# Sliding-window attention with the values as the stationary operand, division after a second transposition, and the router's sums taken head by head

## The chip, the cores and the metric

## The reference

Three stages run one after the other. The attention stage has 2 batches, 8 heads, 768 tokens and 64 columns a head. A token attends to the first 8 keys and to the 96 keys up to itself, with a linear bias for distance:

```
scores = q k^T / 8 - slope[h] * dist ;  a = exp(scores - max) ;  a = a / (sum(a) + 1e-9)
x = concat over heads of (a v)                                   # 2 x 768 x 512
```

The router stage takes `logits = x w_gate` (8 experts) and a gate column `x w_local`. A token whose local gate is below 0.5 takes the best expert, any other takes the expert of the token before it. The token then goes through the two matrices of its expert (512 to 1024 to 512, with a ReLU between them), scaled by its softmax probability.

The mixing stage is a 2-D Fourier transform over tokens and columns, its real part added to the input, a layer norm, and a dense 512 to 2048 to 512 network.

## The kernel before

The kernel is written by hand for each engine with semaphores: the text of an engine is its order of work. The changed part is the attention stage, the branch `windowed > 0`.

**Units.** A unit is one tile of 128 tokens of one pair of heads: 2 batches x 4 pairs x 6 tiles is `UNITS` = 48 units. Unit n belongs to group g = n // 6 (a batch and a pair of heads) and tile i = n % 6. A unit has up to two key tiles of 128 keys for each head (`k` = 0, 1); the first tile of a group (i = 0) has one.

**Loop of TensorE.** Iteration n issues, in this order: `scores(n+2)` (two products of 64 rows with 256 columns, one for each head, on different row halves), `turn(n)` (four transpositions of the probabilities into `prob_t`'s bank), at some steps `turn_x`, at some steps tasks of the router, and then `values(n-1)`. `values` holds a tile of transposed probabilities as the stationary operand and passes 128 columns of the values by it: four products, 8 records, into bank 6. It waits for `x_unit_done`, because VectorE has to have read bank 6.

**Loop of VectorE.** Iteration n: every sixth time `bias_of` (two operations), `scores(n+2)` (scale, bias and maximum, two operations), `turned(n)` (copy of the transposed probabilities out of PSUM), in odd iterations `reciprocals`, at some steps half a piece of `first_rest` (the low part of the first expert's weights), at twelve steps from `STEP_FLAGS` = 34 on a part of the router's work for batch 0 (`stages`: the first of each pair reads bank 6 and waits for `pv_done`, the second stands behind the division), and `normalised(n-1)`, which divides bank 6 into `x_att`.

**Loop of ScalarE.** Iteration n: `exponentials(n+2)` (two Exp, each with its sum), at some steps `copy_x` (transposed x out of bank 7 into `x_t`), and at every fourth step `first_expert` (the high part of a piece of the first expert's weights, 128x1024).

**Router sums.** `turn_x` transposes finished tiles of `x_att` (48 transpositions over the loop), `copy_x` copies them to `x_t`, and `gate_sums` multiplies a tile of `x_t`, held still, by 9 columns of `gate_w`: 48 products for both batches. Batch 0's (`sum_logits`) are tasks of iterations 28 to 33, eight records each. Those of batch 1 are taken in three parts in iterations 40 to 47 and behind the loop.

**After the loop.** `take_logits(1)` on VectorE starts a serial chain: the choice of expert for batch 1, ranks, slots, scatter of x by GpSimd's indirect DMA, load of the sorted tiles by SP. Then TensorE runs the experts and the mixing stage almost without a pause to the end.

**DMA.** SP issues the first loads in one order: `cwin`, keys, `square`, values, `gate_w`, the first weight piece, zeros, then the keys and values of the following groups.

## Time and profile before

| | us |
|---|---|
| median of 3 runs | 662.52 (660.62 to 666.81) |
| the profiled execution, as timed | 663.25 |
| its span in the trace | 661.4 |
| TensorE matmul busy | 641.9 (97%) |
| TensorE weight load busy | 523.3 (79%) |
| VectorE busy | 314.8 (48%) |
| ScalarE busy | 210.0 (32%) |
| GpSimd busy | 213.5 (32%) |

The granted clock of TensorE is 9 tenths or more in all 40 slices, that is 2.4 GHz throughout. PE stands for TensorE's matmuls, PEld for its weight loads, DVE for VectorE, ACT for ScalarE, POOL for GpSimd, SPq for the DMA issues of SyncE. A record of a matmul spans its whole way through the array and overlaps the next one, so the pace of a series is read from start to start and not from the duration.

### The profile page before, as it was taken

How to read it: one execution, taken by the hardware profiler on the slowest of the kernel's cores; microseconds unless marked ns; L12 is line 12 of the kernel's file. 1: busy time of each engine (PE TensorE's matmuls, PEld its weight loads, DVE VectorE, ACT ScalarE, POOL GpSimd, SP SyncE). 2: the span in 40 equal slices, each digit the busy share in tenths (PEclk: the TensorE clock that was granted, in tenths of full speed). 3: DMA queues.
4: the chain of work that ended last, by engine and by line, in shares of the span. 5: the costliest groups of instructions: out<-in, count | busy, mean ns of one | idle time of the engine just before them, and what ended most of it. 6: DMA issues, size and time to landing. Idle time of an engine off the chain costs nothing. (4 is left out here: it accounts for less than half of the span.)

```text
span 661.4 us, 10419 instructions
## 1 busy us (share of the span) xinstructions
PE 641.9 (97%) x3346; PEld 523.3 (79%) x3347; DVE 314.8 (48%) x830; ACT 210.0 (32%) x414; POOL 213.5 (32%) x120
## 2 busy tenths in 40 slices
PE   9999999889999999999998999999999999999997
PEld 7777878768888888887776778888888888888886
DVE  5999787476744544634546864521121112211112
ACT  3566544222444243342215552232111122111110
POOL 0000000233999787987436465340000000000000
PEclk9999999999999999999999999999999999999999
DMA  8897543323777755866444054100010000100001
GB/s 319 301 324 256 209 143 118 113 84 126 249 237 234 264 202 182 282 238 197 151 124 125 1 175 143 35 30 1 1 64 1 0 1 1 63 1 0 1 1 63
DMA packets 36486, 83.71 MB, mean 127 GB/s; under 512 B 3286, under 2 KB 8150, under 8 KB 36440
## 3 DMA queue, kind: packets, MB, share of 16 engines
q1 hardware_dynamic: 19888, 43.34, 18.8%
q10 hardware_dynamic: 14632, 33.46, 15.0%
q0 software_dynamic: 1920, 6.29, 3.0%
q8 instruction: 29, 0.48, 0.3%
q14 instruction: 17, 0.14, 0.1%
HBM read 67.36 MB, written 15.73 MB: 126 GB/s over the span
## 5 line engine op out<-in xcount | busy, mean ns | idle before, releaser
L782 POOL TENSOR_TENSOR w<-raw,w 128x1024 fp32r<-128x1024 f32 x56 | 132.6, 2398 | 26.9 <-ACT w L881 26.9
L1881 DVE SCALAR_TENSOR_TENSOR act_t<-psum,act_t 128x512 fp32r<-128x512 f32 x48 | 33.2, 691 | 190.1 <-ACT act_t L1180 190.1
L881 ACT ACTIVATE w<-raw 128x1024 fp32r<-128x1024 f32 x64 | 67.4, 1058 | 97.2 <-POOL w L782 31.6
L1180 ACT ACTIVATE act_t<-psum 128x512 fp32r<-128x512 f32 x48 | 28.8, 599 | 216.2 <-PE psum L620 216.2
L618 PE MATMUL psum<-un_t,wc 128*128 128x512 f32 x192 | 74.8, 390 | 1.4 <-DVE un_t L1808 1.4
L618 PE MATMUL psum<-wc,act_t 128*128 128x512 f32 x192 | 75.6, 394 | 0.0
L620 PE MATMUL psum<-wc,act_t 128*128 128x512 f32 x192 | 74.9, 390 | 0.0
L619 PE MATMUL psum<-wc,act_t 128*128 128x512 f32 x192 | 74.8, 390 | 0.0
L620 PE MATMUL psum<-un_t,wc 128*128 128x512 f32 x192 | 74.7, 389 | 0.0
L619 PE MATMUL psum<-un_t,wc 128*128 128x512 f32 x192 | 74.7, 389 | 0.0
L954 ACT ACTIVATE prob<-prob,top 128x256 f32<-128x256 f32 (+1 forms) x96 | 46.3, 482 | 51.5 <-DVE top L1521 47.9
L790 POOL DMA_INDIRECT x_sorted<-x_att,slots x12 | 11.8, 987 | 134.7 <-DVE slots L1367 131.6
L618 PE MATMUL psum<-w,xs_t 128*128 (+1 forms) x128 | 52.1, 407 | 1.3 <-POOL w L782 1.0
L618 PE MATMUL psum<-w,hid_t 128*128 (+1 forms) x128 | 51.6, 403 | 0.8 <-DVE hid_t L1684 0.8
L2112 PE MATMUL psum<-v_win,prob_t 128*128 128x128 f32 x352 | 49.2, 281 | 1.8 <-DVE x_att L1549 1.7
L620 PE MATMUL psum<-w,xs_t 128*128 (+1 forms) x128 | 50.2, 392 | 0.0
L620 PE MATMUL psum<-w,hid_t 128*128 (+1 forms) x128 | 50.1, 391 | 0.0
L619 PE MATMUL psum<-w,hid_t 128*128 (+1 forms) x128 | 49.9, 390 | 0.0
L619 PE MATMUL psum<-w,xs_t 128*128 (+1 forms) x128 | 49.8, 389 | 0.0
L862 POOL TENSOR_TENSOR wc<-raw,wc 128x1024 fp32r<-128x1024 f32 x15 | 35.7, 2402 | 31.6 <-ACT wc L1130 24.4
L2112 PEld LDWEIGHTS psum<-v_win,prob_t 128*128 128x128 f32 x352 | 43.0, 192 | 3.5 <-issue 3.4
L618 PEld LDWEIGHTS psum<-un_t,wc 128*128 128x128 f32 x192 | 36.1, 188 | 9.1 <-DVE un_t L1808 1.6
(289 smaller groups left out, 1099.4 us busy)
## 6 DMA issues: line engine op xcount, KB each, us to landing
raw<-in_moe_w ACTq DMA_DIRECT2D x56, 512.0 KB, 4.3
raw<-in_moe_w_ch SPq DMA_DIRECT2D x12, 512.0 KB, 3.3
k_win<-in_k SPq DMA_DIRECT2D x7, 768.0 KB, 7.6
v_win<-in_v SPq DMA_DIRECT2D x7, 704.0 KB, 5.2
xs<-x_sorted SPq DMA_DIRECT2D x17, 256.0 KB, 4.2
raw<-in_moe_w SPq DMA_DIRECT2D x8, 512.0 KB, 8.5
y_sorted<-ys SPq DMA_DIRECT2D x16, 256.0 KB, 3.6
out<-u SPq DMA_DIRECT2D x12, 256.0 KB, 2.0
```

Source lines behind the costliest of these rows:

```text
L618: nc.tensor.matmul(target, left_h, right_h, start=first, stop=False)
L619: nc.tensor.matmul(target, left_h, right_l, start=False, stop=False)
L620: return nc.tensor.matmul(target, left_l, right_h, start=False, stop=last)
L782: nc.gpsimd.tensor_tensor(w[:, slot, 1, m, at_:at_ + PIECE], raw[:, n % RING, :], w[:, slot, 0, m, at_:at_ + PIECE].bitcast(f32), ALU.subt ...
L790: pool.indirect_dma_start(x_sorted[:, :], bass.IndirectOffsetOnAxis(ap=slots[:, t:t + 1], axis=0), x_att[:, t, :], None).then_inc(first_sc ...
L862: nc.gpsimd.tensor_tensor(lo, source, hi.bitcast(f32), ALU.subtract).then_inc(wc_ready, 1)
L881: nc.scalar.activation(w[:, slot, 0, m, at_:at_ + PIECE], raw[:, n % RING, :], ACT.Copy).then_inc(high_done, 1)
L954: ins = nc.scalar.activation(prob[n % 3][:, t, c0:], prob[n % 3][:, t, c0:], ACT.Exp, bias=top[:, n % 3, t:t + 1], scale=-1.0, accum_out=s ...
L1180: nc.scalar.activation(act_t[n % 2][:, 0, :], bank(act_bank(n)), ACT.Relu).then_inc(act_high, 1)
L1881: nc.vector.scalar_tensor_tensor(act_t[n % 2][:, 1, :], bank(act_bank(n)), 0.0, act_t[n % 2][:, 0, :].bitcast(f32), ALU.max, ALU.subtract) ...
L2112: ins = nc.tensor.matmul(bank(6)[:, t * D:t * D + P], prob_t[n % 2][:, 2 * t + k, :], v_flat[r][:, at_:at_ + P], start=(k == k0), stop=(k ...
```

## The change

- `values(n)` holds a tile of the values still (`v_win`) and passes both heads' probabilities by it as 256 columns: two products (4 records) of 256 columns in place of four (8 records) of 128. Bank 6 then holds both heads' values by both heads' probabilities with the head's columns on the partitions; the two quarters that belong together are used. `OVER`, the place of the router's results in bank 6, moves behind the 256 columns.
- ScalarE copies the two quarters into `x_pair` (two copies of 64 partitions x 128 columns a unit, `copy_pair(n-1)` in iteration n, behind `exponentials(n+2)` and ahead of `first_expert`). `values(n)` on TensorE now waits for `pair_copied`, no longer for the division.
- TensorE turns `x_pair` back to tokens (`turn_pair(n-2)` in iteration n, between `turn(n)` and `values(n-1)`: one transposition into bank 7), and multiplies the same tile, held still, by `gate_pair`: 18 columns, the router's 9 sums for each of the two heads.
- VectorE divides from bank 7 (`normalised(n-2)` in iteration n) and once in a group multiplies the group's gate sums by the reciprocals into `by_head`. `add_heads` adds over heads: over 8 in a stage of its own for batch 0, over 6 at iteration 45 for batch 1; `take_logits(1)` adds the last two with two operations.
- `turn_x`, `copy_x`, `sum_logits`, `sum_part`, `sum_third`, `sum_last` leave this branch.
- `STEP_FLAGS` is 28 in place of 34, with one stage more at its head; the bank-reading stages wait for `pair_copied` in place of `pv_done`. `PIECE_STEPS` is every fifth step in place of every fourth.
- One DMA more: `gate_pair` (72 columns, 36 KB) behind `gate_w` on SP's queue, and TensorE waits for both before iteration 0.

The diff, cut to its core (the other branch and the declarations are left out):

```diff
@@ -555,28 +567,24 @@
             return 5 - n % 2
-        X_FILLS = []
-        for g_ in range(B * HP - 2):
-            X_FILLS += [(6 * g_ + 9, g_, 0, 4), (6 * g_ + 10, g_, 4, 2)]
-        X_FILLS += [(41, 6, 0, 4), (43, 6, 4, 2), (45, 7, 0, 2), (47, 7, 2, 2), (UNITS, 7, 4, 2)]
+        X_FILLS = [(g_, t0, n) for g_ in range(B * HP) for t0, n in ((0, 4), (4, 2))]
         def x_fills_for(g, t):
-            return 1 + [t0 <= t < t0 + n and g_ == g for _, g_, t0, n in X_FILLS].index(True)
-
-        PIECE_STEPS = {4 * i + 3: i for i in range(WPIECES)}
-
-        SUM_STEP = {ST * HP + 4 + t: t for t in range(ST)}
-        PART_STEP = {40 + t: t for t in range(ST)}
-        THIRD_STEP = {42 + t: t for t in range(ST)}
-        PART_TAKEN = 46
-        LAST_STEP = 47
-        STEP_FLAGS = 34
+            return 2 * g + 1 + t // 4
+
+        PIECE_STEPS = {5 * i + 3: i for i in range(WPIECES)}
+
+        PART_TAKEN = 45
+        STEP_FLAGS = 28
         small = bank(6)
-        OVER = P + D
+        OVER = 2 * P
         BANK_LOGITS, BANK_PART = (small[:, P + OVER + n * ST * (E + 1):P + OVER + (n + 1) * ST * (E + 1)]
                                   for n in range(2))
         BANK_LAST = bank(7)[:, 2 * P:2 * P + ST * (E + 1)]
+        BANK_PAIR = [bank(7)[:, m * P:(m + 1) * P] for m in range(2)]
+        BANK_GATED = [bank(7)[:, 2 * P + n * 2 * ST * (E + 1):2 * P + (n + 1) * 2 * ST * (E + 1)]
+                      .rearrange("p (i t e) -> p i t e", i=ST, t=2) for n in range(2)]
         BANK_FLAGS = small[0:ST, 2 * P:4 * P]
         BANK_KEEP, BANK_FRESH = small[0:ST, 2 * P:3 * P], small[0:ST, 3 * P:4 * P]
         BANK_ENDS = small[0:1, OVER:OVER + 2 * ST]
...
@@ -657,6 +665,8 @@
                 first_group_keys(p)
                 first_group_values(p)
             sp.dma_start(gate_w[:, :, :], a["gate"]).then_inc(gate_loaded, 16)
+            sp.dma_start(gate_pair[:, :, :, :].rearrange("p c t e -> p (c t e)"),
+                         a["gate_pair"].rearrange("p c t e -> p (c t e)")).then_inc(gate_loaded, 16)
             def first_piece(n):
                 sp.dma_start(raw[:, n, :], w1_d[:, 0:1, n, :].rearrange("p e f -> p (e f)")
                              ).then_inc(raw_loaded[n], 16)
...
@@ -956,19 +966,28 @@
                                                    accum_out=sums[:, n % 4, t:t + 1])
                     ins.then_inc(prob_ready, 1)
+                def copy_pair(n):
+
+                    act.wait_ge(pv_done, n + 1)
+                    if n >= 3:
+                        act.wait_ge(pair_turned, n - 2)
+                    for t in range(2):
+                        rows = slice(t * D, (t + 1) * D)
+                        ins = nc.scalar.activation(x_pair[rows, n % 3, :], bank(6)[rows, t * P:(t + 1) * P], ACT.Copy)
+                    ins.then_inc(pair_copied, 1)
+
                 exponentials(0)
                 exponentials(1)
                 for n in range(UNITS):
                     if n + 2 < UNITS:
                         exponentials(n + 2)
-                    for k, fill in enumerate(X_FILLS):
-                        if fill[0] == n:
-                            copy_x(k)
+                    if n > 0:
+                        copy_pair(n - 1)
                     if n in PIECE_STEPS:
                         first_expert(PIECE_STEPS[n])
-                    if n == STEP_FLAGS + 1:
+                    if n == STEP_FLAGS + 2:
                         gate_exponentials(0)
-                copy_x(len(X_FILLS) - 1)
+                copy_pair(UNITS - 1)
             with nc.scalar.Else():
                 with act.Fori(0, B * HP) as group:
                     for v in range(2 * ST):
...
@@ -1251,15 +1270,20 @@
             def take_logits(b):
+                flat = logits[:, :, :].rearrange("p t e -> p (t e)")
                 if b == 0:
                     dve.wait_ge(logit_sums, ST)
-                    nc.vector.tensor_copy(logits[:, :, :].rearrange("p t e -> p (t e)"), BANK_LOGITS
-                                          ).then_inc(logits_ready, 1)
+                    nc.vector.tensor_copy(flat, BANK_LOGITS).then_inc(logits_ready, 1)
                 else:
-                    dve.wait_ge(last_sums, ST)
-                    nc.vector.tensor_tensor(logits[:, :, :].rearrange("p t e -> p (t e)"), BANK_LAST,
-                                            logits_part[:, :, :].rearrange("p t e -> p (t e)"), ALU.add
+                    link(nc.vector.tensor_tensor(logits_part[:, :, :], logits_part[:, :, :], by_head[:, :, H - 2, :],
+                                                 ALU.add))
+                    nc.vector.tensor_tensor(logits[:, :, :], logits_part[:, :, :], by_head[:, :, H - 1, :], ALU.add
                                             ).then_inc(logits_ready, 1)
+
+            def add_heads(into, heads):
+                return nc.vector.tensor_reduce(into[:, :, :],
+                                               by_head[:, :, 0:heads, :].rearrange("p t h e -> p t e h"),
+                                               AX.X, ALU.add)
             def below_top(b):
                 dve.wait_ge(logits_ready, b + 1)
...
@@ -1537,21 +1561,31 @@
                 def reciprocals(n):
                     both = slice((n - 1) % 4, n % 4 + 1)
-                    nc.vector.tensor_scalar(inv[:, both, :], sums[:, both, :], 1e-9, None, ALU.add
+                    kept = inv_all[:, n - 1:n + 1, :]
+                    nc.vector.tensor_scalar(kept, sums[:, both, :], 1e-9, None, ALU.add
                                             ).then_inc(sums_eps, 1)
                     dve.wait_ge(sums_eps, (n + 1) // 2)
-                    nc.vector.reciprocal(inv[:, both, :], inv[:, both, :]).then_inc(inv_ready, 1)
+                    nc.vector.reciprocal(kept, kept).then_inc(inv_ready, 1)
                 def normalised(n):
                     g, i = n // ST, n % ST
-                    dve.wait_ge(pv_done, n + 1)
+                    dve.wait_ge(pair_turned, n + 1)
                     dve.wait_ge(inv_ready, n // 2 + 1)
+                    if i == ST - 1:
+                        nc.vector.tensor_tensor(
+                            by_head[:, :, 2 * (g % HP):2 * (g % HP) + 2, :], BANK_GATED[g % 2],
+                            inv_all[:, g * ST:(g + 1) * ST, :].unsqueeze(3).broadcast_to([P, ST, 2, E + 1]), ALU.mult
+                            ).then_inc(pair_gated, 1)
                     nc.vector.tensor_tensor(
                         x_att[:, (g // HP) * ST + i, (g % HP) * P:(g % HP + 1) * P].rearrange("p (t d) -> p t d", t=2),
-                        bank(6)[:, 0:P].rearrange("p (t d) -> p t d", t=2),
-                        inv[:, n % 4, :].unsqueeze(2).broadcast_to([P, 2, D]), ALU.mult).then_inc(x_unit_done, 1)
-
-                stages = ((take_logits, below_top), (None, best_codes), (None, choose_fresh),
+                        BANK_PAIR[n % 2].rearrange("p (t d) -> p t d", t=2),
+                        inv_all[:, n, :].unsqueeze(2).broadcast_to([P, 2, D]), ALU.mult).then_inc(x_unit_done, 1)
+
+                def sum_heads(b):
+                    dve.wait_ge(pair_gated, HP)
+                    add_heads(logits, H).then_inc(logits_ready, 1)
+
+                stages = ((None, sum_heads), (None, below_top), (None, best_codes), (None, choose_fresh),
                           (take_flags, run_in_tiles), (take_ends, run_over_tiles), (all_codes, None),
                           (hot_codes, None), (take_counts, rank_all), (None, place), (None, areas),
                           (None, share_sums), (None, share))
...
@@ -1573,19 +1607,19 @@
                     reads_bank, behind = stages[n - STEP_FLAGS] if 0 <= n - STEP_FLAGS < len(stages) else (None, None)
                     if reads_bank is not None:
-                        dve.wait_ge(pv_done, n)
+                        dve.wait_ge(pair_copied, n)
                         reads_bank(0)
+                    if n > 1:
+                        normalised(n - 2)
                     if n == PART_TAKEN:
-                        dve.wait_ge(pv_done, n)
-                        take_part()
-                    if n == LAST_STEP:
-                        dve.wait_ge(pv_done, n)
-                        take_third()
-                    if n > 0:
-                        normalised(n - 1)
+                        dve.wait_ge(pair_gated, 2 * HP - 1)
+                        add_heads(logits_part, H - 2).then_inc(part_ready, 1)
                     if behind is not None:
                         behind(0)
+                normalised(UNITS - 2)
                 normalised(UNITS - 1)
+                dve.wait_ge(part_ready, 1)
+                dve.wait_ge(pair_gated, 2 * HP)
                 chain_end, chain[0] = chain[0], chain_start
             with nc.vector.Else():
                 dve.wait_ge(g_dist, 16)
...
@@ -2095,58 +2134,52 @@
                     g, i, r = n // ST, n % ST, n // ST % 2
                     k0 = 1 if i == 0 else 0
                     pe.wait_ge(prob_t_ready, n + 1)
-
-                    if g == 0 and i == 0:
-                        pe.wait_ge(first_values[0], VALUES_FIRST)
-                    if g == 0 and i % 2 == 1 and i < ST - 1:
-                        pe.wait_ge(first_values[i // 2 + 1], VALUES_FIRST)
+                    if g == 0 and i % 2 == 0:
+                        pe.wait_ge(first_values[i // 2], VALUES_FIRST)
                     if g > 0 and i == 0:
                         pe.wait_ge(v_loaded[r], (VALUES_FIRST if r == 0 else 16) + 16 * (g // 2))
                     if n > 0:
-                        pe.wait_ge(x_unit_done, n)
+                        pe.wait_ge(pair_copied, n)
                     for task in tasks:
                         task()
-                    for t in range(2):
-                        for k in range(k0, 2):
-                            at_ = (2 * i + k - 1) * P + t * D
-                            ins = nc.tensor.matmul(bank(6)[:, t * D:t * D + P], prob_t[n % 2][:, 2 * t + k, :],
-                                                   v_flat[r][:, at_:at_ + P], start=(k == k0), stop=(k == 1))
+                    for k in range(k0, 2):
+                        ins = nc.tensor.matmul(bank(6)[:, 0:2 * P], v_win[r][:, 2 * i + k - 1, :],
+                                               prob_t[n % 2][:, k:4:2, :], start=(k == k0), stop=(k == 1))
                     ins.then_inc(pv_done, 1)
+
+                def turn_pair(n):
+                    g, i = n // ST, n % ST
+                    pe.wait_ge(pair_copied, n + 1)
+                    if n > 0:
+                        pe.wait_ge(x_unit_done, n)
+                    nc.tensor.transpose(BANK_PAIR[n % 2], x_pair[:, n % 3, :], ident)
+                    nc.tensor.matmul(BANK_GATED[g % 2][:, i, :, :].rearrange("p t e -> p (t e)"), x_pair[:, n % 3, :],
+                                     gate_pair[:, g % HP, :, :].rearrange("p t e -> p (t e)"), start=True, stop=True
+                                     ).then_inc(pair_turned, 1)
                 scores(0)
                 scores(1)
                 warm_up(4)
                 pe.wait_ge(square_loaded, 16)
                 pe.wait_ge(v_padded, 2)
-                by_step = {STEP_FLAGS + 3: turn_flags, STEP_FLAGS + 4: ends_to_row, STEP_FLAGS + 5: carry_to_column,
-                           STEP_FLAGS + 6: codes_to_columns, STEP_FLAGS + 7: rank_tokens}
+                pe.wait_ge(gate_loaded, 2 * 16)
+                by_step = {STEP_FLAGS + 4: turn_flags, STEP_FLAGS + 5: ends_to_row, STEP_FLAGS + 6: carry_to_column,
+                           STEP_FLAGS + 7: codes_to_columns, STEP_FLAGS + 8: rank_tokens}
                 for n in range(UNITS):
                     if n + 2 < UNITS:
                         scores(n + 2)
                     turn(n)
-                    for k, (step_, g, t0, size) in enumerate(X_FILLS):
-                        if step_ == n:
-                            pe.wait_ge(x_unit_done, g * ST + t0 + size)
-                            turn_x(k)
+                    if n > 1:
+                        turn_pair(n - 2)
                     tasks = []
-                    if n in SUM_STEP:
-                        tasks.append(lambda t=SUM_STEP[n]: sum_logits(t))
                     if n in by_step:
                         tasks.append(lambda stage=by_step[n]: stage(0))
-                    if n in PART_STEP:
-                        tasks.append(lambda t=PART_STEP[n]: sum_part(t))
-                    if n in THIRD_STEP:
-                        tasks.append(lambda t=THIRD_STEP[n]: sum_third(t))
                     if n > 0:
                         values(n - 1, tasks)
-                for t in (2, 3, 0, 1):
-                    sum_last(t)
+                turn_pair(UNITS - 2)
                 values(UNITS - 1)
-                pe.wait_ge(x_unit_done, UNITS)
-                turn_x(len(X_FILLS) - 1)
                 turn_tile(0, 0, 16)
-                for t in range(4, ST):
-                    sum_last(t)
+                turn_pair(UNITS - 1)
                 keep_busy(5, bank(0))
             with nc.tensor.Else():
                 pe.sem_inc(g_x, 1)
```

## Rows read from the trace of the kernel before

**Rows 1.** The page: the span, and busy time of each engine.

```profile
span 661.4 us, 10419 instructions
PE 641.9 (97%) x3346; PEld 523.3 (79%) x3347; DVE 314.8 (48%) x830; ACT 210.0 (32%) x414; POOL 213.5 (32%) x120
```

**Rows 2.** Windows: stretch, length, then busy (records) of PE, PEld, DVE, ACT, POOL.

```profile
10.78:70.96 60.18, 58.42 (x433) 44.90 (x432) 54.74 (x214) 38.48 (x130) 0.00 (x0) 1.00 0.87 311
70.96:121.01 50.05, 48.78 (x386) 40.34 (x386) 39.25 (x165) 23.17 (x82) 5.05 (x5) 1.00 0.40 142
121.01:132.17 11.16, 8.40 (x64) 7.40 (x63) 4.71 (x18) 2.25 (x7) 0.97 (x1) 1.00 0.22 74
132.17:661.40 529.23, 516.49 (x2411) 421.64 (x2409) 211.04 (x413) 144.12 (x193) 206.32 (x104) 1.00 0.31 102
```

**Rows 3.** Timeline of PE, one plain unit: start, length, line, count of records.

```profile
33.75 0.70 PE L2079 MATMUL psum<-k_win,q_t 64*128 64x256 f32 x4
34.39 0.66 PE L2090 MATMUL psum<-square,prob 128*128 128x128 f32 x4
34.88 1.06 PE L2112 MATMUL psum<-v_win,prob_t 128*128 128x128 f32 x8
35.87 0.70 PE L2079 MATMUL psum<-k_win,q_t 64*128 64x256 f32 x4
```

**Rows 4.** Timeline of PE: filler products of 256 fp32 columns, each with its weight load.

```profile
130.91 2.40 PE L1985 MATMUL psum<-square 128*128 128x256 f32 x10
...
148.67 4.05 PE L1985 MATMUL psum<-square 128*128 128x256 f32 x18
```

**Rows 5.** Groups by line (count, busy, mean ns), and eight gate loads of the timeline.

```profile
L2112 PE MATMUL psum<-v_win,prob_t 128*128 128x128 f32 x352 | 49.2, 281 | 1.8 <-DVE x_att L1549 1.7
...
80.79 0.97 PEld L1933 LDWEIGHTS psum<-gate_w,x_t 128*128 128x128 f32 x8
```

**Rows 6.** Groups of ACT by line and shape: copies out of PSUM, shorter Exp.

```profile
L954 ACT ACTIVATE prob<-prob,top 128x128 f32<-128x128 f32 x16 | 6.3, 394 | 9.8 <-DVE top L1521 9.6
...
L916 ACT ACTIVATE x_t<-psum 128x512 f32<-128x512 f32 x7 | 4.0, 574 | 0.0
L916 ACT ACTIVATE x_t<-psum 128x256 f32<-128x256 f32 x10 | 3.7, 368 | 7.0 <-PE psum L1927 6.1 <-remote 0.9
```

**Rows 7.** Timeline of all engines, 78 to 83 us: who follows whom.

```profile
78.70 1.14 PE L2112 MATMUL psum<-v_win,prob_t 128*128 128x128 f32 x8
...
79.77 0.70 PE L2079 MATMUL psum<-k_win,q_t 64*128 64x256 f32 x4
...
79.88 0.29 DVE L1549 TENSOR_TENSOR x_att<-psum,inv 128x128 f32<-128x128 f32 x1 [1.03 <-PE psum L2112]
...
80.52 0.42 DVE L1521 CUSTOM_DVE_ANT_0 prob<-psum,pair_bias 128x256 f32<-128x256 f32 x1 [0.35 <-PE psum L2079]
...
81.33 0.51 ACT L954 ACTIVATE prob<-prob,top 128x256 f32<-128x256 f32 x1 [1.70 <-DVE top L1521]
...
82.33 1.04 ACT L881 ACTIVATE w<-raw 128x1024 fp32r<-128x1024 f32 x1
```

**Rows 8.** DMA: issue of `gate_w` and of the first piece; `gate_w` to landing.

```profile
6.12 0.44 SPq L659 DMA_DIRECT2D gate_w<-in_gate  x1
...
6.60 0.45 SPq L661 DMA_DIRECT2D raw<-in_moe_w  x1
...
DMA to landing us min/median/max: 5.5/5.5/5.5
```

**Rows 9.** Group of DVE by line and shape: a router step on six partitions.

```profile
L1316 DVE TENSOR_TENSOR_SCAN kept_all<-flags_t,zeros 6x128 f32<-6x128 f32 x2 | 0.8, 386 | 0.0
```

**Rows 10.** Timeline of the end of the attention stage.

```profile
123.88 0.36 PE L1933 MATMUL psum<-gate_w,x_t 128*128 128x9 f32 x2 [2.27 <-DVE prob_t L1535]
...
129.18 0.29 DVE L1549 TENSOR_TENSOR x_att<-psum,inv 128x128 f32<-128x128 f32 x1 [1.31 <-PE psum L2112]
...
132.17 0.21 DVE L1260 TENSOR_TENSOR logits<-psum,logits_part 128x54 f32<-128x54 f32 x1 [2.70 <-issue]
```

23 lines of the change are left out of this document (18 added, 5 removed).

## Prediction

> **What bounds the kernel now.** I read the page first [rows 1]: TensorE's matmul rows cover 97% of the span, VectorE 48%, ScalarE 32%. The windows [rows 2] split this. The loop over 48 units runs from 10.78 to 121.01, its end with the chain to the logits of batch 1 to 132.17, and then 529 us follow in which TensorE is 98% busy and which the change doesn't touch. They move as a whole with the moment of those logits, so only the first 132 us are to be costed. In the first window of the loop (28 units, 60.18 us, 2.15 a unit) VectorE is 91% busy and TensorE idle for 1.8; in the second (18 units, 50.05 us, 2.78 a unit) VectorE is at 78%, TensorE idle for 1.3, and the router's sums are what has been added. TensorE's order of work sets the pace, with VectorE close behind in the first window.
>
> A plain unit shows TensorE's ledger by starts [rows 3]: scores 33.75 to 34.39 (0.64), four transpositions to 34.88 (0.49, of which 0.11 is the first load of the series behind it), eight records of `values` to 35.87 (0.99), in all 2.12.
>
> **The values.** Eight records of 128 columns take 0.99, that is 0.124 each [rows 3]. Records of 256 fp32 columns follow one another at 0.21 with their loads hidden: 18 take 4.05 and 10 take 2.40, so eight more cost 1.65 [rows 4]. Four of them are 0.85 us. Gain: 0.13 a unit, 0.11 where there is one key tile (half the records, estimate); 40 x 0.13 + 8 x 0.11 = 6.1 us over the loop.
>
> The Trainium skill ("Perfetto Trace Analysis", Identifying the Most-Contended Engine) says to judge TensorE's headroom by its weight loads' busy time and not by the matmuls'. By that rule halving the loads would be the gain, and it is a rival below.
>
> **What moves on TensorE.** Transpositions: 48 before, 48 after, nothing. Gate sums: 48 products of 96 records before and after, each bound by its load, 0.11 to 0.12 (eight loads in 0.97 [rows 5]; eight records from 80.90 to the next `values` at 0.1 each). But they move: before, 80 of the 96 records stood in the second window and none in the first; now every unit has 2, 0.22 us. So the ledger per window changes like this. First window, 28 units: +28 x (0.22 - 0.13) = +2.5. Second, 18 units: -80 x 0.11 + 18 x 0.22 - 18 x 0.13 - some 4 transpositions x 0.11 = -7.6.
>
> **ScalarE's copies.** Two copies of 64 x 128 out of PSUM a unit. Rows of 256 and 512 columns take 368 and 574 ns [rows 6]: 0.8 ns a column and 162 ns fixed, so 0.27 for 128 columns, start to start 0.18, both finished 0.45 after the first starts. Lower bound 0.16 each (the fixed part), upper bound 0.39, the Exp of 128 columns [rows 6]; I take 0.27, since those rows are Copy out of PSUM too. ScalarE's load goes from 38.5 to about 50 in the first window: room enough. They lie on a path, though, worked out from [rows 7]. From TensorE's scores (79.77) to VectorE's is 0.75, from there to the first Exp 0.81, both Exp until ScalarE is free 1.00 (81.33 to 82.33), copies 0.45, wake-up 0.06: `pair_copied` comes 3.07 after the iteration's start. `values` started 1.46 after it and is visible 1.08 later (its four records, and the 0.2 by which 79.88 follows the last of the eight of 78.70), at 2.54, just before the Exp are over. `turn_pair` wants it after one period (0.64 + 0.38 + 0.33 + 0.11 + 0.85 = 2.31) and 1.02 more, at 3.33. So a plain unit costs nothing, with 0.26 us to spare. Iterations with one key tile are shorter on TensorE, and one in six waits about 0.1; a VectorE that is late (bias together with half a weight piece, twice in this window) costs 0.5 each time. Waits of the first window after the change: 5 x 0.1 + 2 x 0.5 = 1.5.
>
> Its waits before: six units have a ledger of 6 x 2.12 + 6 x 0.11 for transpositions, less 0.21, 0.22 and 0.45 for the short scores, turn and values (estimates, half of the long ones), 12.5 or 2.08 a unit; 28 x 2.08 less 1.4 for the first units, which have no `values` and no transposition yet, is 56.8, and 60.18 - 56.8 = 3.4 are waits, 1.8 of them plain idle [rows 2]. They come from divisions that VectorE does late, behind its wait for `values(n-1)`. That wait goes: it now divides n-2 out of another bank, and the unit of 2.17 gives it more time. So 56.8 + 2.5 + 0.2 (two transpositions more) + 1.5 = 61.0: **+0.7**. Bounds: -0.8 (no waits) and +5 (half of the late moments of VectorE reach TensorE).
>
> **The five reading stages.** This is the largest term. `take_flags` to `take_counts` (iterations 32 to 36) now wait for `pair_copied(n)`, which stands behind `exponentials(n+2)`, which waits for `scores(n+2)` of VectorE in the same iteration. That closes a ring: VectorE's scores, +0.81 Exp, +1.00, +0.45 copies, +0.06, then the stage, the division, what stands behind it, and only then `scores(n+3)`. One turn is 2.32 + stage + 0.25 + behind. Operations on six partitions cost about 0.39 [rows 9], small ones 0.2 to 0.25 (the 0.21 of [rows 10] and a link). So: flags 2.32 + 0.45 + 0.25 + 0.75 = 3.75; ends 3.1; codes 2.95; hot codes 2.85; counts, with four linked operations behind, 3.9: 16.5 against 5 x 2.17 = 10.9, +5.7. Before, the same stages waited for `pv_done`, without ScalarE in the ring. Around them VectorE is overloaded: `sum_heads` to `choose_fresh` at 29 to 31 together with a weight piece and reciprocals (+1), `place` (1.1 us in an odd iteration) and `share_sums` with bias and a piece (+2). All together +8; less the 0.3 of slack and the 0.7 that TensorE's own idle of 1.3 loses: second window -7.6 + 7.0 = **-0.6**, bounds -7.6 and +4.
>
> **The start.** TensorE now waits for `gate_pair` before iteration 0. SP issues it where the first piece stood, at 6.60, and the transfer before it took 5.5 to land [rows 8], so 12.1 against 10.78: **+1.3**. Lower bound 0.8 (landing in 5.0), upper bound 2.5. The DMAs behind it come 0.45 later; keys of group 1, issued at about 9, are not needed before 19: nothing.
>
> **The end.** From the start of iteration 46 (121.0) each `values` now follows the last through copy and `turn_pair`: 1.08 + 0.45 + 0.06 + 0.11 + 0.33 = 2.03. `values(45)` at +1.15, (46) +3.15, (47) +5.15, `turn_pair(47)` +6.75, seen at +7.3, gate product and division to +7.85. Before, the division of unit 47 began at 129.18, that is +8.2 with a wait of 2.27 before it that no row explains [rows 10]. VectorE then leaves the loop's branch: 2.70 idle until 132.17 though the last sums were there at 131.1 [rows 10]. If that is the cost of the branch's end, it is now fully exposed: +7.85 + 2.7, and one addition more, 0.25: 10.8 against 11.2, **-0.4**. Bounds: -2.0 (only 1.1 of it repeats), +1.9 (a wait of 2.3 as before comes again).
>
> **Sum.** +0.7 - 0.6 + 1.3 - 0.4 = +1.0. The profiled span was 661.4, its run 663.25, the median of three 662.52, 1.1 above the span. So 662.5 + 1.0 = **663.5**. Runs of this kernel can't tell a change under 1% (6.6 us) from none; this is one.
>
> **Rivals.**
> 1. *TensorE's ledger is paid out.* The reading ring doesn't bite, because the stages' work hides in the wait. For it: VectorE's busy falls from 91 to 78% in the second window. Against it: the ring holds only in-order steps that all have rows. It gives 663.5 - 7.5 = 656; with the end at its lower bound 654. Chance 0.14.
> 2. *The copies close a ring in every unit* (slower). If a copy costs 0.39 as the short Exp, the pair ends 0.24 later, and the 0.26 to spare is gone. From there every lateness of VectorE, some 0.25 a unit, goes to TensorE: 40 x 0.22 = 9 us, 672. It decides from 0.40 a copy on, or from 0.25 us of mean lateness. For it: `copy_pair` stands in order behind Exp that wait for VectorE, and VectorE is at 91% in the first window. Against it: rows of copies out of PSUM. Chance 0.21.
> 3. *The loads were the bound.* 176 loads of `values` fewer at 0.12 [rows 5] are 21 us: 641. Against it: fillers of 256 columns go at 0.21 a record [rows 4], though their one load would fit twice into it nearly, so the columns set their pace. By the rule quoted above the loads would set it. Chance 0.02.
>
> My forecast has 0.63, with a range of its own of 659 to 668. The range over all reaches to 656 and to 671. Faster by over 1%: rival 3 and most of rival 1, 0.13. Slower by over 1%: most of rival 2, 0.19. The rest, 0.68, is no change.
>
> **What the changed kernel's profile would show.** Records of `values` at 0.21 from start to start, a plain unit of 2.3; copies of 0.27; the first `scores` of the loop 1.3 later. The first window's 28 units should take about 61, the next 18 units 49.5 with periods of 2.9 to 3.9 in iterations 32 to 36, where VectorE's reading operation waits for ScalarE's copy. A copy of 0.4, many waits of TensorE's `x_pair` load for ScalarE, or periods of 2.3 in iterations 32 to 36 would make this wrong, as would a different cost of the branch's end.

## The result, and the profile after

| | before | after |
|---|---|---|
| median, us | 662.77 (660.62 to 666.81, 4 runs) | 675.25 (672.93 to 677.23, 4 runs) |
| the profiled execution, its span | 661.4 | 670.8 |
| TensorE matmul busy | 641.9 | 645.1 |
| TensorE weight load busy | 523.3 | 510.6 |
| ScalarE busy | 210.0 | 230.5 |

After is 1.018 of before, 95% interval [1.0121, 1.0238]: some 12 us slower, where 1 was forecast and 671 was the upper end of the range.

The windows of after, cut at the same iterations as [rows 2] (stretch, length, then busy and records of PE, PEld, DVE, ACT and POOL, the granted clock, DMA share, GB/s). The first is iterations 0 to 3, which had no window of their own before:

```profile
12.19:21.22 9.03, 9.03 (x47) 5.62 (x47) 6.05 (x26) 5.12 (x19) 0.00 (x0) 0.81 1.01 402
21.22:78.08 56.86, 56.36 (x345) 38.17 (x344) 47.84 (x191) 43.18 (x150) 0.00 (x0) 1.00 0.75 256
78.08:129.69 51.61, 45.06 (x273) 29.89 (x273) 42.06 (x178) 32.03 (x114) 6.45 (x6) 1.00 0.43 154
129.69:141.10 11.41, 8.43 (x47) 6.36 (x45) 3.86 (x13) 2.50 (x10) 0.00 (x0) 1.00 0.01 4
140.00:144.00 4.00, 0.83 (x3) 0.36 (x4) 2.74 (x12) 1.05 (x3) 0.00 (x0) 0.77 0.02 6
144.00:148.00 4.00, 3.51 (x13) 1.79 (x13) 1.56 (x8) 0.00 (x0) 0.00 (x0) 0.50 0.00 0
148.00:152.00 4.00, 3.72 (x11) 3.14 (x12) 2.88 (x15) 0.00 (x0) 0.51 (x1) 0.50 0.00 0
152.00:156.00 4.00, 3.48 (x17) 2.50 (x15) 0.90 (x4) 1.68 (x3) 3.08 (x4) 0.95 0.45 174
```

Iterations whose scores are those of a first tile (records of 64x128 in place of 64x256) mark every sixth iteration in both traces, so that the loss can be put in a ledger. The scores of iteration 4 start at 17.93 before and 21.22 after; those of iteration 28 at 70.96 and 78.08; `turn(46)` at 121.01 and 129.69; the flags' transposition behind the logits at 134.13 and 143.06; the first `hid` of the experts on ScalarE at 140.19 and 152.10.

| stretch | before | after | loss, us |
|---|---|---|---|
| to iteration 4 | 17.93 | 21.22 | +3.3 |
| 4 to 28 | 53.03 | 56.86 | +3.8 |
| 28 to 46 | 50.05 | 51.61 | +1.6 |
| 46 to the flags | 13.12 | 13.37 | +0.3 |
| flags to the first `hid` | 6.06 | 9.04 | +3.0 |
| sum | | | +11.9 |

The rest of the program, which the change leaves alone, took 518.7 in this execution of after and 521.2 in that of before, so the spans differ by only 9.4. In the other kernels of this study that do the same routing it took 519.2 to 524.7; that is scatter (last section), and the 11.9 is close to the 12.5 between the medians.

**A plain unit.** TensorE's timeline (start, length of the group, line, records), to be laid beside [rows 3]:

```profile
23.44 0.70 PE L2118 MATMUL psum<-k_win,q_t 64*128 64x256 f32 x4
24.07 0.66 PE L2129 MATMUL psum<-square,prob 128*128 128x128 f32 x4
24.56 0.29 PE L2155 MATMUL psum<-square,x_pair 128*128 128x128 f32 x1
24.69 0.29 PE L2156 MATMUL psum<-gate_pair,x_pair 128*128 128x18 f32 x2
24.83 1.11 PE L2146 MATMUL psum<-prob_t,v_win 128*128 128x256 f32 x4
25.87 0.49 PE L2118 MATMUL psum<-k_win,q_t 64*128 64x256 f32 x2
```

The unit takes 2.43, where 2.31 was forecast. The scores (0.63) and `turn` (0.49) stand as forecast, and transposition and gate product together (0.13 and 0.14) take less than the 0.33 of the forecast. But the four records of 256 columns take 1.04 from their first to the next scores, where eight of 128 took 0.99 and 0.85 was forecast. The reader sees here the error of the largest saving. An iteration with one key tile has half the records, and the difference of the two kinds gives their true pace:

```profile
29.48 0.68 PE L2146 MATMUL psum<-prob_t,v_win 128*128 128x256 f32 x2
30.09 0.49 PE L2118 MATMUL psum<-k_win,q_t 64*128 64x256 f32 x2
```

Two records take 0.61, four take 1.04: 0.215 a record, and 0.18 that the scores start later than that pace asks for, whatever the number. In the kernel before, eight took 0.99 [rows 3] and four took 0.54:

```profile
38.90 0.61 PE L2112 MATMUL psum<-v_win,prob_t 128*128 128x128 f32 x4
39.44 0.70 PE L2079 MATMUL psum<-k_win,q_t 64*128 64x256 f32 x4
```

That is 0.11 a record, and 0.09 beside it. Two records of 128 columns cost about the same as one of 256 (0.22 and 0.215). What sets the 0.11 can't be told from this: a weight load alone goes at nearly the same pace (eight gate loads in 0.97 [rows 5]).

**The start.** TensorE waits for `gate_pair` until 12.19 and then works at half clock, 1.2 GHz, for part of the next few us (granted clock 0.57 in 12 to 16 us), where before it began at 10.78:

```profile
12.19 1.04 PE L2118 MATMUL psum<-k_win,q_t 64*128 64x256 f32 x4 [1.92 <-issue]
13.16 0.69 PE L2129 MATMUL psum<-square,prob 128*128 128x128 f32 x2
13.77 1.23 PE L2118 MATMUL psum<-k_win,q_t 64*128 64x256 f32 x4
```

The same four records of scores take 1.23 here and 0.70 in the plain unit. The row names no releaser; in two other traces with the same wait (the second run of the changed kernel and the one with fewer gate products) it is the DMA of `gate_pair`.

**The ring.** TensorE's iteration 33 of after, with VectorE still in its 32nd (what released a step is in brackets):

```profile
90.08 0.70 PE L2118 MATMUL psum<-k_win,q_t 64*128 64x256 f32 x4
90.54 0.56 ACT L976 ACTIVATE x_pair<-psum 64x128 f32<-64x128 f32 x2
...
91.13 0.41 DVE L1335 COPY flags_t<-psum 6x256 f32<-6x256 f32 x1 [1.13 <-ACT x_pair L976]
91.57 0.29 DVE L1579 TENSOR_TENSOR x_att<-psum,inv_all 128x128 f32<-128x128 f32 x1
...
92.01 0.30 PE L2155 MATMUL psum<-square,x_pair 128*128 128x128 f32 x1 [0.64 <-DVE x_att L1579]
```

VectorE waits for the copies, the division follows, and TensorE's transposition waits for the division. The next scores follow at 93.87, a period of 3.79; the following three start after another 3.21, 3.52 and 3.02.

**A gap that not every execution has.** In iterations 41 and 42 both ScalarE (until 117.24) and VectorE (until 118.84) stand still for something that the trace calls only "remote" (rows of the waits of 20 to 130 us: total, times, longest):

```profile
DVE prob L1545 <- remote: 1.5, 1, 1.5
ACT x_pair L976 <- remote: 1.0, 1, 1.0
```

Iteration 40 to `turn(46)` takes 16.94 here. In the runs below with more fillers and with the last unit moved, whose loops up to there are the same, neither row is there and it takes 15.40 and 15.41. So 1.5 us of the 51.61 belong to this execution and not to the change. No run shows the cause.

**The end.** VectorE's last rows of the loop, and the first behind it, to be laid beside [rows 10]:

```profile
137.33 0.27 DVE L1575 TENSOR_TENSOR by_head<-psum,inv_all 128x108 f32<-128x108 f32 x1 [1.77 <-PE psum L2156]
137.52 0.28 DVE L1579 TENSOR_TENSOR x_att<-psum,inv_all 128x128 f32<-128x128 f32 x1
140.85 0.22 DVE L1278 TENSOR_TENSOR logits_part<-logits_part,by_head 128x54 f32<-128x54 f32 x1 [3.05 <-issue]
143.06 0.37 PE L1996 MATMUL psum<-square,keep_old 128*6 128x128 f32 x1 [3.52 <-DVE fresh L1319]
```

TensorE, whose five filler products (ten records) end at 139.54, is idle for 3.52, and the windows above show half clock from about 143 to 152. Before it was idle for 0.81 there, at full clock.

### The profile page after: what moved, and what is told of

The parts are those of the page before. It is cut to its first block, busy times and chain, and to the rows that moved or that the text cites. A ratio compares the mean times of both kernels' runs of the same rounds, so it can differ in the third digit from the quotient of the medians.

```text
span 670.8 us, 10221 instructions
## 1 busy us (share of the span) xinstructions
PE 645.1 (96%) x3170; PEld 510.6 (76%) x3171; DVE 316.0 (47%) x838; ACT 230.5 (34%) x493; POOL 214.3 (32%) x120
## 4 chain that ended last, share of the span: by engine, by line
PE 83%; DVE 8%; issue 4%; ACT 2%; DMA 1%; POOL 0%; another core or an unknown queue 0%; DVEq 0%; SPq 0%; ACTq 0%; POOLq 0%
PE psum L626 22%; PE psum L628 22%; PE psum L627 22%; PE psum L2146 4%; PE psum L2118 3%; PE psum L2129 2%; PE psum L2078 2%; DVE prob L1545 1%; PE psum L2155 1%; PE psum L2031 1%; ACT x_pair L976 1%; ACT prob L964 1%; PE psum L2320 1%; DVE prob_t L1559 1%; PE psum L2024 1%
## 5 line engine op out<-in xcount | busy, mean ns | idle before, releaser
L626 PE MATMUL psum<-w,xs_t 128*128 (+1 forms) x128 | 53.3, 417 | 0.1
L628 PE MATMUL psum<-w,xs_t 128*128 (+1 forms) x128 | 51.1, 400 | 0.0
L627 PE MATMUL psum<-w,xs_t 128*128 (+1 forms) x128 | 50.8, 397 | 0.0
L2146 PE MATMUL psum<-prob_t,v_win 128*128 128x256 f32 x176 | 49.7, 401 | 0.0
L1545 DVE CUSTOM_DVE_ANT_0 prob<-psum,pair_bias 128x256 f32<-128x256 f32 (+1 forms) x96 | 34.6, 399 | 16.6 <-PE psum L2118 14.2
```

Source lines behind the costliest of these rows:

```text
L626: nc.tensor.matmul(target, left_h, right_h, start=first, stop=False)
L627: nc.tensor.matmul(target, left_h, right_l, start=False, stop=False)
L628: return nc.tensor.matmul(target, left_l, right_h, start=False, stop=last)
L1545: ins = nc.vector.tensor_tensor_reduce(out=prob[n % 3][:, t, c0:], in0=bank(2 * (n % 2) + t)[:, c0:KW], in1=pair_bias[:, t, m0:m0 + KW - c ...
L2146: ins = nc.tensor.matmul(bank(6)[:, 0:2 * P], v_win[r][:, 2 * i + k - 1, :], prob_t[n % 2][:, k:4:2, :], start=(k == k0), stop=(k == 1))
```

## Experiments

All are edits of the changed kernel. A ratio is to the kernel before, run beside it on the same chip. The changed kernel itself, run again:

> The changed kernel unaltered, on the chip of the runs beside it, as their yardstick. Expected 1.018 times the kernel before, 674 to 677 us, with a span of 671 to 675; a clock at half between about 12 and 16 us and between about 140 and 152 us.

Measured 676.35 (673.26 to 681.18), 1.0191 [1.0117, 1.0264]. The scores of iteration 4 came at 22.76 (after: 21.22), since the half clock lasted longer, 0.50 in 12 to 16 and 0.67 in 16 to 20. From iteration 4 to 28 it took 56.85, and from the flags to `hid` 9.04, as in the first execution of the changed kernel, "after" from here on.

**The wait for `gate_pair` moved to where it is first read.**

```diff
                 pe.wait_ge(v_padded, 2)
-                pe.wait_ge(gate_loaded, 2 * 16)
...
                     pe.wait_ge(pair_copied, n + 1)
+                    if n == 0:
+                        pe.wait_ge(gate_loaded, 2 * 16)
```

> The changed kernel with the wait for the two gate tables moved from ahead of the loop to the first multiplication by them (iteration 2). Theory: the wait costs 1.4 us itself and, through TensorE's idle time of 1.9 us after which the clock was granted at half, some 1.9 more: 3.3 us less than the changed kernel, first scores of iteration 4 at about 18 in place of 21.2. Rival (only the wait counts, the slow first iterations have another cause, such as loads that share the DMA engines): 1.4 us less, and the records between 12 and 16 us stay slow.

**The wait kept, and twelve warm-up products ahead of it in place of four.**

> The changed kernel with the wait left ahead of the loop, but twelve warm-up products in place of four before it, so that TensorE is busy while it waits. Theory (the clock is half of the loss): the wait of 1.4 us stays, the clock stays at full, 1.5 to 2 us less than the changed kernel. Rival (the slow records come from the late tables or loads): no difference to the changed kernel.

Measured: 673.19 (1.014 [1.0063, 1.0216]) for the first and 673.21 (1.0133 [1.0077, 1.0189]) for the second, against 676.35 on the same chip. The scores of iteration 4 came at 18.02 and 20.12, against 22.76 and the 17.93 of before. With the warm-up products TensorE was idle for 0.38 ahead of the loop, in place of 1.92, and the clock stayed at 1.00:

```profile
12.19 0.70 PE L2118 MATMUL psum<-k_win,q_t 64*128 64x256 f32 x4 [0.38 <-issue]
```

So the start has two parts: the wait itself is 2.1 (20.12 less 18.02), and the half clock that it brings is 1.1 (in after) to 2.6 (in the run here). The late wait removes both. The ratios' intervals overlap; it is the traces that separate these. The half clock doesn't come every time: of the nine traces with this wait and four warm-up products, seven have it, behind 1.92 to 2.82 of idle time, and two don't, behind 1.11 (more fillers at the end) and 1.59 (other banks). Those two reach iteration 4 at 19.89 and 19.87, about where the twelve warm-up products do.

**Products of 256 columns split again into two of 128, the values still held.**

```diff
-                    for k in range(k0, 2):
-                        ins = nc.tensor.matmul(bank(6)[:, 0:2 * P], v_win[r][:, 2 * i + k - 1, :],
-                                               prob_t[n % 2][:, k:4:2, :], start=(k == k0), stop=(k == 1))
+                    for t in range(2):
+                        for k in range(k0, 2):
+                            ins = nc.tensor.matmul(bank(6)[:, t * P:(t + 1) * P], v_win[r][:, 2 * i + k - 1, :],
+                                                   prob_t[n % 2][:, 2 * t + k, :], start=(k == k0), stop=(k == 1))
```

> The changed kernel with each product of 256 columns taken apart into two of 128 (one per head), with the same result: 8 records and 8 weight loads a unit in place of 4 and 4. By the prediction's price (0.124 us for a record of 128 columns, 0.21 for one of 256) this costs 0.13 us a unit, 6 us more than the changed kernel. Theory now: the columns set the pace in both forms (0.11 and 0.215 a record) and what differs is the gap until the next scores, which is shorter after narrow records: 0 to 0.06 us a unit less, 0 to 3 us less in all. A unit's values, from their first record to the next scores, 0.99 in place of 1.04.

Measured 676.13, against 676.35 unsplit; 1.0161 [1.011, 1.0213]. Its unit, in the same view as above:

```profile
26.30 1.14 PE L2147 MATMUL psum<-prob_t,v_win 128*128 128x128 f32 x8
27.37 0.49 PE L2118 MATMUL psum<-k_win,q_t 64*128 64x256 f32 x2
...
31.00 0.69 PE L2147 MATMUL psum<-prob_t,v_win 128*128 128x128 f32 x4
31.62 0.49 PE L2118 MATMUL psum<-k_win,q_t 64*128 64x256 f32 x2
```

1.07 for eight and 0.62 for four, beside 1.04 and 0.61. Twice the records and twice the loads cost 0.01 to 0.03 a unit, and iterations 4 to 28 took 57.17 beside 56.85. This settles the price of the values: the fewer, wider records bring next to nothing. The Trainium skill ("Perfetto Trace Analysis", Identifying the Most-Contended Engine) judges TensorE's headroom by MFU (the share of its peak arithmetic that is used) and its weight loads' busy time. Here the loads' busy time fell by 12.7 us while the kernel became slower, and putting 176 loads back changed no time. As a price of a load, which is how the third rival used it, that busy time is of no use in this loop.

**Thirteen fillers at the end in place of five.**

> The changed kernel with thirteen filler products behind the loop in place of five, 3.4 us more of work that nobody waits for, ending before the flags of batch 1 are ready. Theory (the idle time of 3.5 us in which VectorE leaves the loop's branch costs a clock at half for the next 8 to 10 us): the clock stays at full, about 3 us less than the changed kernel. Rival (the chain there hangs on VectorE and not on TensorE's clock): no difference.

Measured 669.57, 1.0171 [1.0129, 1.0213]. The clock stays at 1.00 throughout 140 to 160, and from the flags to `hid` it takes 6.04 (139.94 to 145.98), as before the change (6.06), where after takes 9.04. The traces give the clock's price at the end as 3.0 us. The ratio hardly moves from the 1.0191 of the unaltered kernel on another chip, and with its interval it can't show the gain on its own.

**The copies of a unit ahead of the Exp.**

```diff
+                    if n > 0:
+                        copy_pair(n - 1)
                     if n + 2 < UNITS:
                         exponentials(n + 2)
-                    if n > 0:
-                        copy_pair(n - 1)
```

> The changed kernel with ScalarE's copies of unit n-1 ahead of the exponentials of unit n+2 instead of behind them. Theory (a ring: VectorE's scores, Exp, copies, the router stage that waits for the copies, the next scores): the Exp leave the ring, iterations 32 to 36 fall from 3.1 to 3.8 us to about 2.5 to 3.0, and the 18 units that took 51.6 us take about 47; 3 to 5 us less in all. Rival (VectorE's load by itself is what stretches these units, or the exponentials now come late): less than 1 us less, or more time.

Measured 674.22, 1.0209 [1.0179, 1.024]: no gain. The marks say why. Iterations 28 to 40 took 32.88 in place of 34.67, but 4 to 28 took 58.29 in place of 56.86: TensorE waited there for 2.0 in all, each time for the division, where it had waited for 0.4 for a copy. The likely reason is that the Exp now come late and everything behind them. The ring got only 0.35 shorter a turn (3.44 and 2.86 for iterations 33 and 34, where after has 3.79 and 3.21 for the same work). What TensorE still waits for in 78 to 130 is nearly all the division (the other 0.4 us are two waits for router steps):

```profile
PE psum L2155 <- DVE x_att L1579: 3.4, 8, 0.9
```

So there were two rings, one nearly as long as the other. Through Exp: scores, Exp, copies, stage, division. And without them: `values`, copies, stage, division, `turn_pair`, `values`. The prediction had only the first. Breaking it brings what lies between the two.

**The last gate product and division moved behind the end of VectorE's branch.** (The same lines, called after `If`/`Else` have joined; a semaphore is kept level for the general branch.)

> The changed kernel with VectorE's last gate product and division behind the end of the loop's branch instead of ahead of it, so that leaving the branch runs while unit 47 is still copied and turned. The other branch isn't kept right here. Theory (leaving the branch costs about 3 us wherever it stands, and was exposed): the logits of batch 1 come about 2.7 us earlier, TensorE's idle time there falls from 3.5 to under 1 us, the clock stays at full, so 5 to 6 us less in all. Rival (the 3.05 us are a wait of another kind, such as for the sums or for late instructions that any place meets): the gap moves along, no gain.

Measured 668.8, 1.0137 [1.0116, 1.0157]. VectorE is idle as long as before, but now while TensorE and ScalarE finish the last unit:

```profile
136.71 0.27 DVE L1531 TENSOR_TENSOR by_head<-psum,inv_all 128x108 f32<-128x108 f32 x1 [2.77 <-issue]
```

From `turn(46)` to the flags it takes 11.22, against 13.37 in after and 13.1 to 13.3 in the other traces with the old end and all gate products: 2.15 us less, where 2.7 was expected. (From iteration 40 it takes 26.63 against 30.31, but 1.5 of that is the gap of iterations 41 and 42, which this execution doesn't have.) The idle time belongs to leaving the branch, wherever the work stands; of its 2.77, 1.0 still comes behind the end of TensorE's last product of the unit, at 135.67. TensorE is idle for 1.37 in place of 3.52, the clock falls all the same (0.60 in 144 to 148), for a shorter time, and flags to `hid` takes 7.28.

**Late wait, copies first and the late last unit together.**

> The three repairs together: gate tables awaited at their first use, copies ahead of the exponentials, last division behind the branch. If the three causes are separate, the gains add: 3.2 (measured) + 4 + 5.5, 12 to 13 us less than the changed kernel, about 663 us or 0.998 of the kernel before. If they share a cause, less.

Measured 663.57, 1.0072 [1.0051, 1.0094], clock 1.00 in all of its span. That is some 8 us less than the changed kernel (1.0191), where 12 to 13 were expected. By the marks, against after, the start gave 3.0, the end 5.3 (11.03 to the flags and 6.06 to `hid`), and the copies 0.4 (58.29 and 32.89 for the two stretches) where 4 was expected. Here TensorE is idle for 1.32 ahead of the flags and the clock stays full, so the idle time alone doesn't say whether it falls.

**The router's results of batch 0 in other banks.** The kernel keeps ScalarE and VectorE out of one PSUM bank at a time: a stage that reads bank 6 stands behind the copies out of it. Now the results are put in the upper halves of banks 2 and 0, whose lower halves hold scores of the other parity (the fillers' output moves to bank 1):

```diff
-        BANK_FLAGS = small[0:ST, 2 * P:4 * P]
+        even, odd = (bank(2), small), (bank(0), small)
+        BANK_FLAGS = [x[0:ST, 2 * P:4 * P] for x in even]
...
-                        dve.wait_ge(pair_copied, n)
                         reads_bank(0)
...
                 for n in range(UNITS):
+                    if n - 1 in by_step:
+                        pe.wait_ge(x_unit_done, n - 2)
                     if n + 2 < UNITS:
                         scores(n + 2)
```

> The router's results of batch 0 are put in the unused halves of the scores' banks 0 and 2, which ScalarE never touches, so the reading stages of iterations 32 to 36 no longer wait for the copies; TensorE waits for their division before the next scores. Theory (these stages stand in a ring through values, copy, stage, division, turn back, of which copying first took away only one side): VectorE's waits for ScalarE's copies (4.1 us in 78 to 130 of the changed kernel) go, iterations 28 to 40 take 32 to 33 us in place of 34.7, the whole 1.5 to 2.5 us less than the changed kernel. Rival (VectorE's own load of 2.9 to 3.4 us in these iterations sets their length): 34 to 34.7 and less than 0.7 us in the whole.

Measured 671.64 (1.0107 [1.007, 1.0144]), against 676.92 (1.0141 [1.0074, 1.0207]) for the changed kernel beside it; the intervals overlap, and the marks decide. Iterations 28 to 40 took 32.22, within the 32 to 33 of the theory of the ring. VectorE waits for no copy any more in 78 to 130, where in after it waited for them for 4.1 in all. What it waits for is scores (and 1.6 for the gap of iterations 41 and 42, which this execution has):

```profile
DVE prob L1546 <- PE psum L2117: 4.2, 5, 1.3
```

So the ring cost 2.5 us in these iterations. 32.22 is also what the kernel before took for them (32.20: 70.96 to 103.16), though that had its batch-0 sums there as well.

**The gate product left out for groups 2 to 7.**

```diff
+                    if g < 2:
+                        ins = nc.tensor.matmul(BANK_GATED[g % 2][:, i, :, :] ...
```

> The gate product of turn_pair is left out for groups 2 to 7 (iterations 14 to 49), whose sums then repeat those of groups 0 and 1, so that the tokens go to other experts than in the reference. Theory (TensorE's order sets the pace, and two records of 0.11 a unit are 0.22 on it): iterations 14 to 28 take 14 x 0.22 = 3.1 us less, so 4 to 28 take 53.8 in place of 56.86; 28 to 46 about 2 less, as far as VectorE's own work lets it; the whole 4 to 6 us below the changed kernel. Rival (the products run under waits that come anyhow): 4 to 28 at 56.5 or more, the whole less than 1 us below.

Iterations 4 to 28 took 55.47 (23.09 to 78.56) in place of 56.85: 1.4 less where 14 x 0.22 = 3.1 was expected, and 28 to 40 took 34.41, 0.3 less. A unit without the product can take 1.99, but the next one then waits for a copy:

```profile
51.27 0.49 PE L2118 MATMUL psum<-k_win,q_t 64*128 64x128 f32 x4
51.69 0.66 PE L2129 MATMUL psum<-square,prob 128*128 128x128 f32 x4
52.19 0.27 PE L2155 MATMUL psum<-square,x_pair 128*128 128x128 f32 x1
52.30 1.03 PE L2146 MATMUL psum<-prob_t,v_win 128*128 128x256 f32 x4
53.26 0.70 PE L2118 MATMUL psum<-k_win,q_t 64*128 64x256 f32 x4
53.89 0.66 PE L2129 MATMUL psum<-square,prob 128*128 128x128 f32 x4
54.57 0.33 PE L2155 MATMUL psum<-square,x_pair 128*128 128x128 f32 x1
```

The transposition starts 0.50 after `turn` in the first unit and 0.68 in the second, where the copy it waits for ends at 54.52. With the product the same two units took 2.21 and 2.44. Both theories missed: the product is 0.22 on TensorE, but only 0.1 a unit comes back, since right beneath lies the path through Exp and copies that rival 2 described (waits of TensorE for copies in 44 to 78: 1.1, in after 0.4). Its whole time (692.16) can't be read, because the routing differs and the experts' part with it.

**The best of these together:** late wait, late last unit, other banks, Exp ahead of the copies.

> Gate wait late, last division behind the branch end and the router's results in banks 0 and 2, together, and the exponentials ahead of the copies as in the change. Theory: first scores of iteration 4 at 18.0; 4 to 28 in 56.9 (58.3 with copies first); 28 to 40 in 32.5; from the last unit to the flags as in the earlier combination; clock full at the end. 2 us less than that combination, so 1.004 of the kernel before (1.000 to 1.008). Rival (VectorE's load sets the reading iterations): 34.5 for 28 to 40 and 1.007 or more.

> The changed kernel unchanged, as a measure for the three others on this chip: 1.018 to 1.019 of the kernel before, iteration 4 to 28 in 56.9 and 28 to 40 in 34.7 us.

Measured: 666.24 (12 runs) and 1.0009 [0.9981, 1.0038] of before, beside the 676.92 of the changed kernel. Marks: iteration 4 at 18.32, 4 to 28 in 56.86, 28 to 40 in 32.22, 40 to the flags in 27.29, flags to `hid` 7.31 with the clock still at 0.64 in 138 to 142. Its time can't be told from that of the kernel before; `hid` comes 1.8 us later (142.00 against 140.19). The 3.8 us of the first window are all still there, and the shorter end (27.29 against the 30.97 of before) pays for most of them; of those 30.97, 2.27 are the wait in iteration 46 that the prediction found no row for, so how much the change itself gains there is open. A kernel faster than before wasn't found.

## Why the prediction was wrong, step by step

**First window, +0.7 forecast: wrong by the price of the values.** The step that failed is "Eight records of 128 columns take 0.99, that is 0.124 each" [rows 3]. Dividing a series' time by its number put the gap ahead of the next scores into the pace, while the fillers' 0.21 [rows 4] was a pace taken between two series of different length. The same subtraction on the values gives 0.11 for 128 columns, that is the 0.21 of 256, and no gain. Without the saving of 28 x 0.13 = 3.6, the +0.7 of the 28 iterations becomes +4.3, that is 3.7 for the 24 from iteration 4 on, and +3.8 was measured in those. Two smaller errors go against each other: transposition and gate product took 0.27 and not 0.33, and the four wide records stand 0.18 and not 0.09 ahead of the scores. TensorE's idle time fell to 0.50 (56.86 less 56.36), from 1.74 in the same iterations before.

**The copies: right in size, their waits too high.** Two took 0.56 as a group of one engine, done 0.59 after the first starts at the stage that waits for them (90.54 to 91.13), where 0.51 was forecast. In the first window TensorE waited for them once, 0.4 in all, where the sum had 1.5 of waits. Rival 2 was wrong as a price of the change, but its ring lies just below, as the run with fewer gate products showed. Cheaper values would then have come back only in part as well; that is argued, no run made the values cheaper.

**The reading ring: right in place and nearly in size.** Periods of 3.79, 3.21, 3.52 and 3.02 of TensorE's iterations 33 to 36 (VectorE's 32 to 35) stand beside forecast turns of 3.75, 3.1, 2.95 and 2.85; bias and a weight piece in the third were counted apart. The turn with the counts, forecast at 3.9, came as 2.31 and then 3.88, the linked operations falling into the next one. The window took 51.61 where 49.45 was forecast; without 18 x 0.13 = 2.3 of the values the forecast would have been 51.8. That these agree is partly luck: 1.5 of the 51.61 is the gap of iterations 41 and 42, which nobody forecast, and without it the same loop took 50.06 and 50.07, so the other terms of this window were 1.7 too high. That ScalarE was its only cause was too simple, as the copies put first showed; moving the results to another bank took it away.

**The start: the wait right, its consequence missed.** Forecast 12.1, measured 12.19 (11.94 to 12.90 in the other traces with this wait). That TensorE is idle for 1.92 there, and then runs at half clock, was not in the sum: +3.3 at iteration 4, not +1.3. Of the 2.0 missed, 0.9 are the wait itself (with the clock full, iteration 4 comes 1.9 to 2.2 behind the kernel before) and 1.1 the half clock.

**The end: right in length, its consequence missed.** The branch end, taken as 2.70 and fully exposed, measured 3.05, and the stretch to the flags +0.3 against -0.4. But with the branch end exposed, TensorE's fillers run out 3.5 us ahead of the next product, and the clock falls to half for some 9 us: +3.0.

So, of the 10.9 us between the forecast (+1.0) and the ledger (+11.9), 5.5 are the values (42 units of 0.13), 2.0 the start, 3.0 the clock at the end and 0.7 the stretch to the flags; the second window came out 0.2 better than the corrected forecast, or 1.7 better and 1.5 worse by the gap.

## What to carry to other kernels

Take the pace of a series of matmuls from two series of different length, never from one series divided by its number; here that alone turned a saving of 6 us into none. Where a change puts a wait on TensorE, look at what the engine does just before and behind it, and price the work behind at both clocks. When a ring of waits is broken, look for the next one through the same buffers before counting the gain; in this loop two rings lay within 0.35 us a turn.

## What the runs showed of the hardware

**Leaving this branch leaves VectorE idle for 2.6 to 3.1 us.** 2.70 before, 3.05 after, 2.77 with a unit moved behind it. In twelve of the fourteen traces (2.70 to 3.05) no releaser is named; in the two combinations the rows of 2.72 and 2.61 name a record of TensorE. In the two gaps looked at (129.4 to 132.2 before, 137.5 to 141 after) the DMA's rows show two and three packets of the queues of kind "instruction"; those of after:

```profile
q8 instruction: 2, 0.03, 3.4%
q14 instruction: 1, 0.01, 0.5%
```

That fits code being loaded for the branch's target, as the Trainium skill has it ("Runtime: NRT & Kernel Launch", Instruction fetch mechanics: a taken branch out of the loaded pages waits for a fetch). No run separated the fetch from the rest, so it stays a likely cause.

**In the mixing stage the clock's half level comes in some executions and not in others.** In five of the fourteen profiled executions the clock stood at half for some 10 us between 366 and 390 us (windows of the stretch), in a part that all kernels share. In the kernel with the copies first:

```profile
370.00:375.00 5.00, 3.46 (x13) 3.04 (x14) 2.92 (x6) 4.58 (x10) 4.12 (x5) 0.61 0.18 50
375.00:380.00 5.00, 5.00 (x20) 4.09 (x19) 4.41 (x10) 2.53 (x3) 5.00 (x5) 0.50 0.00 0
380.00:385.00 5.00, 5.00 (x17) 4.45 (x18) 4.83 (x16) 1.40 (x5) 1.63 (x2) 0.53 0.00 0
```

From the first `hid` to the end these five took 523.4 to 524.7, and the others that do the same routing 518.7 to 521.9. Two of those others, the kernel before and the one with the late wait, have a shorter stretch at half level (0.50 in 362 to 365 before, 0.71 in 360 to 365 with the late wait); they took 521.2 and 521.9. So the clock before isn't at full throughout, though each of the forty slices of its page shows 9 tenths. In the five the fall comes within some 3 us behind TensorE's wait for VectorE's `cos_spec`, which lasted 1.07 to 1.82 there. In the last combination that wait lasted 1.32 and the clock stayed full, so again its length alone doesn't decide.

This is most of the scatter of that stretch. In the loop the gap of iterations 41 and 42 adds to it: nine of the thirteen traces of the changed kernel and its variants have such a "remote" wait there. The four without take 15.4 to 15.5 from iteration 40 to `turn(46)`, and those with one 16.2 to 20.3, but for the kernel with fewer gate products (a wait of 0.6, and 15.2). That is why stretches between marks told more here than medians.
